# Moving the chunk-recurrence steps by one dense group: levels at groups 0, 3, 5, 8 of ten, preparation ahead of the near sums, six weight splits later

## The chip, the cores and the metric

One core of a Trainium2 chip. The time is device microseconds of one launch of the kernel. The kernel before took 1499.67 us in the median of three runs (1497.66 to 1500.48). The execution that was profiled took 1501.16 us; the span of its records is 1499.0 us. TensorE's granted clock has two levels, 1.2 and 2.4 GHz; the mean granted clock of this execution was 0.994 of full speed.

## The reference

Three parts, one after the other, all in float32:

```python
# 1: gated linear attention, B=4, H=8, S=768, D=48
for t in range(S):
    state = alpha[:, :, t, :, None] * state + k[:, :, t] (outer) v[:, :, t]
    y[:, :, t] = einsum('bhd,bhde->bhe', q[:, :, t], state)
x = y.transpose(0, 2, 1, 3).reshape(3072, 384)
# 2: gated layer, d_ff 1536
x = (sigmoid(x @ w_gate) * (x @ w_val)) @ w_out
# 3: four experts of width 1024, each over all tokens
p = domain_probs / domain_probs.sum(-1)
out = sum(p[:, e] * (relu(x @ w1[e]) @ w2[e]) for e in range(4))
```

The recurrence over t is replaced by chunks of 128 tokens. Every float32 product of parts 2 and 3 is made of three products of halves (high x high, high x low, low x high), so each operand is split into a high half, a copy rounded by ScalarE, and a low half, the difference, which VectorE or GpSimd computes.

## The kernel before, in words

**Steps.** A step (`sc`) is one chunk of 128 tokens of one batch entry, 24 in all. Its work on TensorE is a sequence of tasks. Six levels (`LVL`, level 0 to 5, products of K columns with the Q columns in `QX`, L565, at the last level L568) double the reach within the chunk: 16 matmuls of 64 columns each, at level 5 eight. Then come a transpose of k (`TRK`, L573), the output and state products (`YOUT`, `STATE`, L584 to L596) and a transpose of y (`TRX`, L601), which makes the chunk a part of the next dense tile's input. Between two levels of one step lies a chain: VectorE multiplies Q and K by decays (`move_on`, L882) once the level's products are done; ScalarE copies Q columns into `QX` for the next level (`spread_heads`, two instructions of L772); then TensorE may run the next level. For levels 0 to 2 VectorE also keeps the products (L937), for levels 3 to 5 ScalarE does (L743, L749, ahead of its copies of L772).

**Preparation.** Before level 0 of a step VectorE runs `prepare` (L891, L893, L897: a product of decays, and Q and K multiplied), then ScalarE `spread_heads(..., 0)`. GpSimd computes the further decays (L1074) from the result of L891. The task `PREP` stands for this. Each step's inputs (`A`, `KQ`) are loaded by SyncE's queue (L481, L482) into one of two buffers once the step before the last is done with it (`y_done`, `state_done`, `y_near_ready`).

**Near terms.** Beside the levels, GpSimd multiplies rows (`near_products`, L1081 to L1084), VectorE sums them (`near_sums`, L909), and GpSimd makes a part of the output of them (`near_terms`, L1091, L1097), which VectorE adds to y (L947). The row loads of the next step wait for the near terms.

**Dense tiles.** Part 2 runs over 8 tiles of 384 tokens. A tile is a list of 36 groups of nine matmuls of 384 columns, in the order gate f, value f, out f-1. Behind a gate group ScalarE takes the sigmoid (L785), behind a value group VectorE multiplies (L974), ScalarE takes the high half (L789) and GpSimd the low half (L1114), which the out group of the same f needs.

**The order.** Every engine walks the same list: `attention_slots` puts the tasks of the next tile's three steps into the slots of the groups, and each engine does its part of a slot's tasks ahead of its part of the group. In tiles 2 to 7 task number n of 12 stands at group n * 30 // 12, that is at 0, 2, 5, 7 of every ten groups: level 3 of the running step at 0 (with `PREP` of the next), level 4 with the next step's level 0 at 2, level 5 with level 1 at 5, y, state and the next step's level 2 at 7, `TRX` two groups behind. In the first tile (`FIRST_SLOTS`) the tasks stand at every second group. The last tile has no steps. The first three steps run ahead of the first tile (`FIRST`). Banks of the accumulation memory are given out in turn over the same order of tasks.

**Weights of part 2.** The nine pieces n (gate, value, out for each third of the width) are loaded at the start and split: high halves on ScalarE (`high_raw1`, L820, 128x1536), low halves on GpSimd for n = 0 to 2 and 6 to 8 (L1130, L1136), on VectorE for n = 3 to 5 (L989, one third or fourth of a piece at a time). The second third of the weights is needed from gate 4 (group 9 of the first tile) on, the last from gate 8 (group 21) on. ScalarE splits pieces 3 to 5 between the tasks of `FIRST`, and pieces 6 to 8 behind groups 3, 5, 7 of the first tile; VectorE's ten parts stand behind groups 0 to 9, GpSimd's ten behind groups 2, 4, ... 20.

Part 3 starts at about 700 us and uses neither steps nor these splits.

Of the kernel before, what the change touches and what calls it, by code (L numbers as in the profile page):

```python
# [38 lines left out]
CHUNKS = S // C  # L39
# [11 lines left out]
STEPS_T = T1 // C  # L51
# [21 lines left out]
PREP = "prepare"  # L73
AHEAD = 3
ATT_GROUPS = 30


def attention_slots(first_tile):


    slots = [[] for _ in range(ATT_GROUPS + 3)]
    lead = AHEAD if first_tile else 0

    def at(n):
        return 2 + 2 * (n + lead) if first_tile else n * ATT_GROUPS // (4 * STEPS_T)

    if first_tile:
        slots[0].append((PREP, 0, 0))
    for n in range(lead):
        slots[at(n - lead)].append((LVL, 0, n))  # L90
    for n in range(4 * STEPS_T):
        tasks = []
        for j in range(STEPS_T + 1):
            level = n - 4 * j + AHEAD
            if level == LEVELS:
                tasks += [(YOUT, j, 0), (STATE, j, 0)]
        for j in range(STEPS_T + 1):
            level = n - 4 * j + AHEAD
            if 0 <= level < LEVELS:
                tasks.append((LVL, j, level))  # L100
            if level == 0:
                slots[at(n) - 2].append((PREP, j, 0))
            if level == LEVELS - 1:
                slots[at(n) + 1].append((TRK, j, 0))
            if level == LEVELS:
                slots[at(n) + 2].insert(0, (TRX, j, 0))
        slots[at(n)] += tasks
    return slots
# [29 lines left out]
def buffer_of(i, sc):  # L138

    return sc if is_first(i, sc) else sc % 2  # L140
# [95 lines left out]
def attention_moe_program(nc, qk, alpha, v, rows, w_gate, w_val, w_out, probs, w1, w2, masks, eye, out):  # L236
    with ExitStack() as ctx:
# [483 lines left out]
        def _(act):  # L721
            def task(i, base, kind, j, level):
# [2 lines left out]
                if not in_use(kind, sc) or not exists(i, sc):  # L725
                    return
                if kind == PREP:
                    spread_heads(i, sc, 0)
                    return
                bank = PS[:, att_bank0 + bank_of((kind, j, level), base), :]  # L730
                if kind == LVL and level >= MASKED:
# [30 lines left out]
            def spread_heads(i, sc, level):  # L762


                p = buffer_of(i, sc)
                if level == 0:
                    act.wait_ge(prep_ready, per_step(i, sc, 1, 1))
                else:
                    act.wait_ge(kq_ready[p], per_level(i, sc, level - 1))
                for g, rows in enumerate((slice(0, D), slice(HB, HB + D))):  # L770
                    right = level_columns(KQ[p][rows, 0], level)
                    done = nc.scalar.activation(QX[p][rows, :, g, :].rearrange("d a (n t) -> d a n t", t=2 << level), right, ACT.Copy)  # L772
                done.then_inc(qx_ready[p], 1)

            def next_columns(i, base, kind, j, level):


                if kind == LVL and level < LEVELS - 1 and exists(i, base + j):
                    spread_heads(i, base + j, level + 1)

            def group(i, tc, kind, f):
                if kind == "gate":
# [13 lines left out]
            def tile(i, tc, attend=True, follow=True, between={}, ahead=None):  # L796
                slots = slots_of(i, tc) if attend else []
                for n, (kind, nxt, f) in enumerate(dense_groups(follow)):
                    if ahead and (kind, f) == ("out", FC1 - 1):
                        ahead()  # L800
                    for t in slots[n] if n < len(slots) else []:
                        task(i, STEPS_T * (tc + 1), *t)
                    for t in slots[n] if n < len(slots) else []:
                        next_columns(i, STEPS_T * (tc + 1), *t)
                    group(i, tc + nxt, kind, f)
                    if n in between:
                        between[n]()
# [11 lines left out]
                act.wait_ge(raw1_in[n % RAW1], 16 * (n // RAW1 + 1))  # L819
                nc.scalar.activation(weight_parts(n)[0], raw_piece(n), ACT.Copy).then_inc(weight_high, 1)  # L820

            high_after = {(LVL, 0, 2): 0, (LVL, 0, 3): 1, (LVL, 0, 4): 2, (STATE, 0, 0): 3, (TRX, 0, 0): 4, (STATE, 1, 0): 5}
            spread_heads(0, 0, 0)
            spread_heads(0, 1, 0)
            for t in FIRST:
# [5 lines left out]
                    high_raw1(high_after[t])  # L831
            group(0, 0, "gate", 0)
            group(0, 0, "value", 0)
            tile(0, 0, between={2 * n - 9: (lambda n=n: high_raw1(n)) for n in (6, 7, 8)})
            tile(0, 1)
            with act.Fori(1, B - 1) as i:
                tile(i, 0)
# [29 lines left out]
        def _(dve):  # L867
# [44 lines left out]
            def task(i, base, kind, j, level):  # L912
                sc = base + j
                p, chunk = buffer_of(i, sc), sc % CHUNKS
                if not in_use(kind, sc) or not exists(i, sc):
                    return
                if kind == PREP:
                    prepare(i, sc, 0)
                    prepare(i, sc, 1)
                    return  # L920
                bank = PS[:, att_bank0 + bank_of((kind, j, level), base), :]
                if kind == LVL:
# [15 lines left out]
                                            bank.rearrange("s (g n r) -> s g n r", g=H, r=r)).then_inc(level_kept[p], 1)  # L938
                    if is_first(i, sc):
                        first_decays(sc, level)  # L940
                    if base and level == 3:
                        near_sums(i, sc)
                elif kind == YOUT:
                    wait_count(dve, trx_done, per_step(i, sc, 1, 0))
                    dve.wait_ge(y_near_ready, per_step(i, sc, 1, 1))
# [63 lines left out]
                    near_sums(0, sums_after[t])  # L1009
            group(0, 0, "value", 0)  # L1010
            parts = [(n, k) for n in (3, 4, 5) for k in range(THIRD if n == 5 else KD)]
            tile(0, 0, between={at: (lambda n=n, k=k: low_part1(n, k)) for at, (n, k) in enumerate(parts)})

            dve.wait_ge(prob_in, 16)
            dve.tensor_reduce(psum_e[:], prob[:], AX.X, ALU.add).then_inc(prob_step, 1)
# [48 lines left out]
        def _(pool):  # L1064
# [114 lines left out]
            near_products(0, STEPS_T)  # L1179
            group(0, 0, "value", 0)  # L1180
            parts = [(n, k) for n in (6, 7, 8) for k in range(THIRD if n == 8 else KD)]
            tile(0, 0, between={2 + 2 * at: (lambda n=n, k=k: low_part1(n, k)) for at, (n, k) in enumerate(parts)})
            tile(0, 1)
            with pool.Fori(1, B - 1) as i:
                tile(i, 0)
# [76 lines left out]
```

## Time and profile before

| | |
|---|---|
| median of three runs | 1499.67 us |
| profiled execution, its span | 1501.16 us, 1499.0 us |
| TensorE busy | 1435.9 us, 96% of the span |
| VectorE, ScalarE, GpSimd busy | 603.1, 501.4, 583.6 us |
| start-up (first three steps) | 0 to 52 us |
| part 2 with steps beside it | 52 to about 650 us |
| part 3 | from about 700 us |

The busy shares of the slower engines say little: they work in short chains between the matmuls. What counts is where TensorE stands still, so the views below are its waits and the timeline of single steps. Ends of matmuls are modelled and overlap the next start, so distances between starts are the better measure.

### The profile page before, as it was taken

The page shows a single profiled execution, that of the slowest core. Times are in us where ns is not written, and L with a number is a line of the kernel's source. Part 1 is how long each engine was busy: PE and PEld are TensorE (multiplying, and loading weights), DVE is VectorE, ACT ScalarE, POOL GpSimd, SP SyncE. Part 2 cuts the span into 40 slices and gives each one's busy share as a digit, 9 for nine tenths or more (in the row PEclk, how much of TensorE's full clock was granted, in tenths as well). Part 3 has the DMA queues.
Part 4 walks back from the last instruction along what each step waited for, and adds up shares of the span by engine and source line. Part 5 has one row for each costly group of instructions (what it writes and reads, how often), then busy time and mean ns, then how long its engine had stood idle before and what let it go on. Part 6 is the DMA issues. An engine that isn't in the chain of part 4 may idle for free.

```text
span 1499.0 us, 25799 instructions
## 1 busy us (share of the span) xinstructions
PE 1435.9 (96%) x10296; PEld 1324.3 (88%) x10296; DVE 603.1 (40%) x933; ACT 501.4 (33%) x975; POOL 583.6 (39%) x552
## 2 busy tenths in 40 slices
PE   4889999999999999999999999999999999999999
PEld 4888898998889998999999999999999999999998
DVE  7665554536454545312333333333333333333333
ACT  6654534445444445322222222222222222222220
POOL 6574544534454435254423313323234133242120
PEclk9999999999999999999999999999999999999999
DMA  8322221212121212100001001010010010100011
GB/s 302 113 77 76 82 70 51 94 58 83 52 70 51 101 51 83 43 22 22 0 1 43 0 1 42 0 42 1 0 42 0 0 42 0 42 0 0 17 46 63
DMA packets 31109, 70.65 MB, mean 47 GB/s; under 512 B 5168, under 2 KB 14128, under 8 KB 31024
## 3 DMA queue, kind: packets, MB, share of 16 engines
q1 hardware_dynamic: 31024, 69.43, 13.6%
q8 instruction: 64, 1.05, 0.3%
q14 instruction: 21, 0.17, 0.0%
HBM read 64.70 MB, written 4.72 MB: 46 GB/s over the span
## 4 chain that ended last, share of the span: by engine, by line
PE 89%; DVE 4%; ACT 3%; issue 2%; DMA 1%; SPq 0%; DVEq 0%; ACTq 0%
PE PS L671 27%; PE PS L661 27%; PE PS L617 18%; PE PS L627 9%; PE PS L565 4%; ACT QX L772 2%; PE PS L588 2%; DVE near L909 1%; PE PS L584 1%; DVE KQ L897 1%; DMA raw<-in_w_gate 1%; PE PS L568 1%; DVE KQ L882 1%; PE PS L573 1%; DVE TOT L891 0%
## 5 line engine op out<-in xcount | busy, mean ns | idle before, releaser
L1145 POOL TENSOR_TENSOR XS_0l<-x2T,XS_0h 128x1536 fp32r<-128x1536 f32 x24 | 84.5, 3523 | 263.3 <-ACT XS_0h L815 263.3
L1035 DVE SCALAR_TENSOR_TENSOR acc<-PS,prob,acc 128x384 f32<-128x384 f32 x192 | 118.6, 618 | 161.8 <-PE PS L671 161.8
L1145 POOL TENSOR_TENSOR XS_1l<-x2T,XS_1h 128x1536 fp32r<-128x1536 f32 x23 | 80.8, 3514 | 252.4 <-ACT XS_1h L815 252.4
L772 ACT ACTIVATE QX<-KQ 48x256 f32<-48x256 f32 x288 | 120.4, 418 | 151.1 <-DVE KQ L882 103.3
L856 ACT ACTIVATE H_1h<-PS 128x512 fp32r<-128x512 f32 x96 | 57.5, 599 | 311.7 <-PE PS L661 311.7
L856 ACT ACTIVATE H_0h<-PS 128x512 fp32r<-128x512 f32 x96 | 57.3, 600 | 299.4 <-PE PS L661 299.3
L1043 DVE SCALAR_TENSOR_TENSOR H_1l<-PS,H_1h 128x512 fp32r<-128x512 f32 x96 | 66.4, 692 | 197.0 <-ACT H_1h L856 197.0
L1043 DVE SCALAR_TENSOR_TENSOR H_0l<-PS,H_0h 128x512 fp32r<-128x512 f32 x96 | 66.1, 691 | 188.8 <-ACT H_0h L856 188.8
L565 PE MATMUL PS<-QX,KQ 112*64 112x64 f32 x1920 | 81.7, 237 | 56.3 <-ACT QX L772 55.8
L565 PEld LDWEIGHTS PS<-QX,KQ 112*64 112x64 f32 x1920 | 71.8, 148 | 70.5 <-issue 41.0
L882 DVE TENSOR_TENSOR KQ<-KQ,TOT 112x512 f32<-112x512 f32 (+1 forms) x126 | 103.0, 840 | 75.4 <-PE PS L565 48.7
L974 DVE TENSOR_TENSOR hid<-PS,hid 128x384 f32<-128x384 f32 x96 | 53.4, 557 | 164.6 <-PE PS L617 144.4
L1114 POOL TENSOR_TENSOR hs1l<-hid,hs1h 128x384 fp32r<-128x384 f32 x48 | 51.9, 1082 | 130.1 <-ACT hs1h L789 130.1
L1114 POOL TENSOR_TENSOR hs0l<-hid,hs0h 128x384 fp32r<-128x384 f32 x48 | 53.4, 1113 | 106.7 <-ACT hs0h L789 106.7
L785 ACT ACTIVATE hid<-PS 128x384 f32<-128x384 f32 x96 | 47.2, 492 | 80.1 <-PE PS L617 79.1
L937 DVE COPY_PREDICATED AT<-mask,PS 128x512 f32<-128x512 int32 x72 | 65.9, 916 | 0.5
L671 PE MATMUL PS<-W_0l,H_1h 128*128 128x384 f32 x192 | 65.0, 339 | 0.0
L671 PE MATMUL PS<-W_0h,H_0l 128*128 128x384 f32 x192 | 64.9, 338 | 0.0
L671 PE MATMUL PS<-W_0h,H_1l 128*128 128x384 f32 x192 | 64.9, 338 | 0.0
L671 PE MATMUL PS<-W_0l,H_0h 128*128 128x384 f32 x192 | 64.8, 338 | 0.0
L671 PE MATMUL PS<-W_1l,H_0h 128*128 128x384 f32 x192 | 64.8, 337 | 0.0
L671 PE MATMUL PS<-W_0h,H_0h 128*128 128x384 f32 x192 | 64.8, 337 | 0.0
(157 smaller groups left out, 4117.0 us busy)
## 6 DMA issues: line engine op xcount, KB each, us to landing
row<-in_rows SPq DMA_DIRECT2D x24, 768.0 KB, 4.4
KQ<-in_qk SPq DMA_DIRECT2D x24, 448.0 KB, 4.3
V<-in_v SPq DMA_DIRECT2D x24, 384.0 KB, 4.9
rawA<-in_w SPq DMA_DIRECT2D x8, 768.0 KB, 4.6
rawB<-in_w SPq DMA_DIRECT2D x8, 768.0 KB, 6.3
A<-in_alpha SPq DMA_DIRECT2D x24, 224.0 KB, 2.8
out_y<-acc SPq DMA_DIRECT2D x5, 768.0 KB, 3.5
raw<-in_w_gate SPq DMA_DIRECT2D x3, 768.0 KB, 13.2
```

The lines of the kernel that those rows point to most:

```text
L565: mm = pe.matmul(dst[mine, :, right], KQ[p][0:R, 1, a, mine], cols[:, :, right], start=True, stop=True)
L617: mm = pe.matmul(PS[:, bank, 0:T1], W[w][:, n, f * P:(f + 1) * P], xT[p][x][:, n, :], start=(n == 0 and (w, x) == SPLITS[0]), stop=(n == K ...
L627: mm = pe.matmul(PS[:, out_bank0 + n, 0:T1], WO[w][:, f, n * P:(n + 1) * P], hs[f % 2][x][:], start=(f == 0 and (w, x) == SPLITS[0]), stop ...
L661: mm = pe.matmul(PS[:, hidden_banks[f], :], W1[c // TILES2][w][:, n, f * P:(f + 1) * P], XS[c % 2][x][:, n, :], start=(n == 0 and (w, x) = ...
L671: mm = pe.matmul(PS[:, result_banks[u], 0:DM], H2[c % 2][x][:, f, u * P:(u + 1) * P], W2[c // TILES2 % 2][w][:, f, :], start=(f == 0 and ( ...
L772: done = nc.scalar.activation(QX[p][rows, :, g, :].rearrange("d a (n t) -> d a n t", t=2 << level), right, ACT.Copy)
L856: nc.scalar.activation(H2[c % 2][0][:, f, :], PS[:, hidden_banks[f], :], ACT.Relu).then_inc(rh_ready, 1)
L882: dve.tensor_tensor(x, x, y, ALU.mult).then_inc(kq_ready[p], 1)
L1035: dve.scalar_tensor_tensor(out=acc[:, n, :], in0=PS[:, result_banks[u], 0:DM], scalar=weight, in1=acc[:, n, :], op0=ALU.mult, op1=ALU.add) ...
L1043: dve.scalar_tensor_tensor(out=low, in0=PS[:, hidden_banks[f], :], scalar=0.0, in1=high.bitcast(F32), op0=ALU.max, op1=ALU.subtract).then_ ...
L1114: nc.gpsimd.tensor_tensor(hs[f % 2][1][:], hid[f % 2][:], hs[f % 2][0][:].bitcast(F32), ALU.subtract).then_inc(hl_ready, 1)
L1145: nc.gpsimd.tensor_tensor(XS[c % 2][1][:], x2T[:, :, at:at + T2], XS[c % 2][0][:].bitcast(F32), ALU.subtract).then_inc(xsl_ready, 1)
```

## The change

The positions of the twelve task numbers in tiles 2 to 7 become 0, 3, 5, 8 of every ten groups. `PREP` keeps its slot there and in the first tile, but the work behind it changes place: ScalarE's copies for the next step's level 0 move behind all tasks of the slot and behind the running step's copies for level 4, and VectorE's near sums of the running step move from ahead of `prepare` to behind it. The high halves of pieces 3 to 8 are all made in the first tile, behind groups 1, 3, 5, 7, 9, 11; VectorE's parts stand behind groups 2 to 11, GpSimd's behind groups 9, 10, 11, 13, 14, 15, 17, 18, 19, 20.

```diff
     def at(n):
-        return 2 + 2 * (n + lead) if first_tile else n * ATT_GROUPS // (4 * STEPS_T)
+        return 2 + 2 * (n + lead) if first_tile else n // 4 * (ATT_GROUPS // STEPS_T) + (0, 3, 5, 8)[n % 4]
...
             if level == 0:
-                slots[at(n) - 2].append((PREP, j, 0))
+                slots[at(n - 1)].append((PREP, j, 0))
...
@@ ScalarE @@
                 if kind == PREP:
-                    spread_heads(i, sc, 0)
                     return
...
                 if kind == LVL and level < LEVELS - 1 and exists(i, base + j):
                     spread_heads(i, base + j, level + 1)
+                elif kind == PREP and exists(i, base + j):
+                    spread_heads(i, base + j, 0)
...
-            high_after = {(LVL, 0, 2): 0, (LVL, 0, 3): 1, (LVL, 0, 4): 2, (STATE, 0, 0): 3, (TRX, 0, 0): 4, (STATE, 1, 0): 5}
+            high_after = {(LVL, 0, 2): 0, (LVL, 0, 3): 1, (LVL, 0, 4): 2}
...
-            tile(0, 0, between={2 * n - 9: (lambda n=n: high_raw1(n)) for n in (6, 7, 8)})
+            tile(0, 0, between={2 * n - 5: (lambda n=n: high_raw1(n)) for n in range(3, 9)})
...
@@ VectorE @@
+                if kind == PREP:
+                    if exists(i, sc):
+                        prepare(i, sc, 0)
+                        prepare(i, sc, 1)
+                    if not (isinstance(i, int) and CHUNKS * i + sc == STEPS_T):
+                        near_sums(i, sc - 1)
+                    return
                 if not in_use(kind, sc) or not exists(i, sc):
-                    return
-                if kind == PREP:
-                    prepare(i, sc, 0)
-                    prepare(i, sc, 1)
                     return
...
-                    if base and level == 3:
-                        near_sums(i, sc)
...
-            tile(0, 0, between={at: (lambda n=n, k=k: low_part1(n, k)) for at, (n, k) in enumerate(parts)})
+            tile(0, 0, between={at: (lambda n=n, k=k: low_part1(n, k)) for at, (n, k) in enumerate(parts, 2)})
...
@@ GpSimd @@
-            tile(0, 0, between={2 + 2 * at: (lambda n=n, k=k: low_part1(n, k)) for at, (n, k) in enumerate(parts)})
+            tile(0, 0, between={9 + at + n - 6: (lambda n=n, k=k: low_part1(n, k)) for at, (n, k) in enumerate(parts)})
```

## Rows read from the trace of the kernel before

**Rows 1.** Busy time by stretch: stretch, its length, TensorE busy (instructions), granted clock, DMA share, GB/s.
```profile
145.00:650.00 505.00, 475.99 (x4738) 0.99 0.19 66
700.00:1499.00 799.00, 796.09 (x3992) 1.00 0.05 18
```

**Rows 2.** TensorE's waits, 52 to 145 and 145 to 650 us: total us, times, longest.
```profile
PE PS L565 <- ACT QX L772: 7.7, 5, 2.3
...
PE PS L565 <- ACT QX L772: 28.5, 17, 1.8
```

**Rows 3.** Timeline of TensorE: start, duration, then the idle time before and its releaser.
```profile
79.19 1.42 PE L565 MATMUL PS<-QX,KQ 112*64 112x64 f32 x32 [2.31 <-ACT QX L772]
...
102.33 1.15 PE L565 MATMUL PS<-QX,KQ 112*64 112x64 f32 x32 [2.15 <-ACT QX L772]
...
125.64 1.15 PE L565 MATMUL PS<-QX,KQ 112*64 112x64 f32 x32 [2.30 <-ACT QX L772]
```

**Rows 4.** Timeline of TensorE: first dense matmul behind a level 3.
```profile
231.37 0.44 PE L617 MATMUL PS<-xT0h,WGh 128*128 128x384 f32 x1
```

**Rows 5.** Chain of waits: two dense groups on end (start, us, what).
```profile
239.27 3.12 PE PS L617 x18
```

**Rows 6.** Timeline of VectorE in the same step.
```profile
231.49 0.69 DVE L882 TENSOR_TENSOR KQ<-KQ,TOT 112x512 f32<-112x512 f32 x1 [1.56 <-PE PS L565]
232.10 0.94 DVE L909 TENSOR_REDUCE near<-row 128x16 f32<-128x768 f32 x1
232.96 0.41 DVE L891 TENSOR_TENSOR TOT<-A 112x256 f32<-112x256 f32 x1
...
233.90 0.62 DVE L897 TENSOR_TENSOR KQ<-KQ,TOT 112x256 f32<-112x256 f32 x1
```

**Rows 7.** Timeline of ScalarE in the same step.
```profile
231.95 1.09 ACT L749 ACTIVATE AT<-PS 16x128 f32<-16x128 f32 x4
234.55 1.73 ACT L772 ACTIVATE QX<-KQ 48x256 f32<-48x256 f32 x4 [1.51 <-DVE KQ L897]
```

**Rows 8.** Timeline of ScalarE ahead of the first tile's first pair.
```profile
74.38 1.47 ACT L820 ACTIVATE WOh<-raw 128x1536 fp32r<-128x1536 f32 x1
75.76 1.09 ACT L749 ACTIVATE AT<-PS 16x128 f32<-16x128 f32 x4
```

**Rows 9.** TensorE by stretch, from the start of three pairs on: columns as in rows 1.
```profile
102.33:108.30 5.97, 5.97 (x50) 0.71 0.00 0
...
201.23:208.77 7.54, 7.54 (x60) 0.77 0.47 158
...
236.33:242.32 5.99, 5.99 (x59) 1.00 0.01 3
```

**Rows 10.** Level 2 of a step on TensorE, and ScalarE's copies for its level 3.
```profile
543.76 0.65 PE L565 MATMUL PS<-QX,KQ 112*64 112x64 f32 x16
...
547.04 0.85 ACT L772 ACTIVATE QX<-KQ 48x256 f32<-48x256 f32 x2 [5.33 <-DVE KQ L882]
```

**Rows 11.** Behind a pair: copies at 236.33's, moves and copies at 79.19's.
```profile
238.68 1.72 ACT L772 ACTIVATE QX<-KQ 48x256 f32<-48x256 f32 x4
...
79.98 4.32 DVE L882 TENSOR_TENSOR KQ<-KQ,TOT 112x512 f32<-112x512 f32 x2 [1.78 <-PE PS L565]
...
84.33 0.85 ACT L772 ACTIVATE QX<-KQ 48x256 f32<-48x256 f32 x2 [0.58 <-DVE KQ L882]
```

**Rows 12.** Level 2 behind the state, the load's issue, and its landing (page, part 6).
```profile
249.12 0.65 PE L565 MATMUL PS<-QX,KQ 112*64 112x64 f32 x16
...
249.99 0.33 SPq L482 DMA_DIRECT2D KQ<-in_qk  x1
...
KQ<-in_qk SPq DMA_DIRECT2D x24, 448.0 KB, 4.3
```

**Rows 13.** GpSimd by stretch in the first tile, and its weight parts (groups by line).
```profile
76.80:102.00 25.20, 18.11 (x24) 0.93 0.23 76
...
L1136 POOL TENSOR_TENSOR WVl<-raw,WVh 128x512 fp32r<-128x512 f32 x3 | 3.8, 1284 | 0.0
```

## The prediction

> **What bounds the kernel now.** I read the busy time by stretches first. From 700 us to the end TensorE is busy for 796.09 of 799.00 us: nothing the diff touches can be won there, that part only starts earlier or later. From 145 to 650 us, the tiles in which attention steps run beside the dense layers, it is busy for 475.99 of 505.00, so 29.0 us are idle [rows 1]. Next come the waits of TensorE: 28.5 of those 29.0 us are one kind, 17 waits of L565 (the level products) for the ScalarE copies of L772 (QX), none longer than 1.8; the first tile has five more of that kind, 7.7 us [rows 2]. The timeline shows where: always the pair of 32 matmuls, level 4 of the running step and level 0 of the next. In the first tile these pairs waited 2.31, 2.15 and 2.30 [rows 3].
>
> Then one such step in full. The 16 matmuls of level 3 start in group 0 and the dense matmuls behind them at 231.37 [rows 4]. A group of nine takes 1.56 us (18 in 3.12) [rows 5], so two groups end at 234.49; the pair starts only at 236.33, where the last window of [rows 9] begins. On VectorE meanwhile: move_on of level 3 (L882) at 231.49, the near sums (L909) at 232.10, then the three operations of prepare, the first at 232.96, the last at 233.90 and done at 234.52 [rows 6]. ScalarE ends its level 3 copies at 233.04, idles 1.51 us for prepare, and runs four copies of L772 from 234.55 to 236.28 [rows 7]: first two for the next step's level 0, then two for the running step's level 4. The chain is level 3, near sums, prepare, next step's copies, own copies, level 4. It is a latency chain that two groups of dense work don't cover.
>
> **The change part by part.** The numbers 0 to 35 are dense groups of a tile.
>
> Three groups instead of two behind level 3 (groups 0 to 3, 10 to 13, 20 to 23), near sums behind prepare, own copies first. In the step above: three groups end at 231.37 + 3 x 1.56 = 236.05. Prepare starts where the near sums did, 232.10, and lasts as before 1.56 (232.96 to 234.52), so it ends at 233.66 [rows 6]. The copies of L772 take 1.73 / 2 = 0.865 a step [rows 7]: the running step's run from 233.04 to 233.91, the next step's to 234.77. Both are in by 236.05 with 1.3 us to spare, and the second is only needed half a pair later (1.15 / 2 = 0.58 [rows 3]). All 17 waits go: **-28.5 us**. What hides the chain then is the third dense group; without it, the other two edits alone would bring 0.86 (near sums, by the starts 232.10 and 232.96), 0.865 and 0.58, 2.3 in all, against a wait of 1.8 at most, so they too nearly do it. The wait has two covers.
>
> In the first tile the distance stays two groups; only near sums and order change, worth those 2.3 us. The waits of 2.15 and 2.30 go: -4.45. The one of 2.31 at 79.19 goes in part, because there ScalarE is late itself: a weight copy (L820) runs until 75.85 and the level 3 copies until 76.85 [rows 8]. The own copies then end at 77.7 where TensorE comes at 79.19 - 2.31 = 76.88, and the next step's at 78.6 where the first half of the pair ends at 78.3: 0.85 + 0.3 remain, **-1.15**. Together -5.6.
>
> The clock. Four times the granted clock fell behind such a wait, from 2.4 to 1.2 GHz for a part of the window: twice in the first tile (the one from 102.33, 0.71 granted, stands for both) and twice later (that from 201.23, 0.77 granted, for both: 7.54 us passed for what takes 5.99 at 1.00) [rows 9]. Each costs 1.55 us. Ahead of each, TensorE had stood idle for the wait. Of the later two both go, -3.1. Of the first tile's, the one at 102.33 goes, -1.55; the one at 79.19 I leave, as a wait is left there. Bounds: 0 and -6.2.
>
> What is shortened. Level 4 to level 5 has groups 3 to 5, two where it had three; level 2 to level 3 has 8 to 10, two for three. Level 2 first, one of its latest rows: the level 2 products start at 543.76, and ScalarE has the copies for level 3 at 547.04 + 0.85 = 547.89, 4.13 later [rows 10]. The products (0.65), two groups (3.12) and the transposes of y (0.25, an estimate: three matmuls twice as wide as the sixteen of 0.65) cover 4.02. The excess is 0.11. It applies at 12 places (two in each of six tiles; behind the third stands the tile's end). Allowing for a few later ones I take **+0.5** in all; the upper bound, 19, is worked out under rival 2. Level 4 to 5: the level 1 copies behind the pair of 236.33 end at 240.40, 4.07 after its start [rows 11]; there are 1.15 + 3.12 and 0.5 for level 5, which goes ahead of level 1: 4.8. I take 0, upper bound 20 by the same rival.
>
> The next step's inputs. PREP of group 10 refills a buffer that is free once Y and STATE of group 8 (before: 7) are done. Its KQ load was issued at 249.99, 0.9 behind the state products (level 2 follows them at 249.12), and a load lands after 4.3 us (median) [rows 12]: 5.2 behind them. Prepare will come level 2, two groups, transposes, level 3 and move_on later, 0.65 + 3.12 + 0.25 + 0.65 + 0.69 = 5.36. So this transfer, hidden before, becomes just hidden, and a delay of up to 1.3 us more is taken by the spare time above. Cost 0, upper bound a few tenths for each of 12 places. SyncE's queue issues nothing else in another order. On GpSimd decays, near terms and near products keep their order; each is released earlier relative to its step. VectorE's gating product (hid) of group 7 now stands ahead of the Y work rather than behind it, which can only help the output groups.
>
> The weights. Three ScalarE copies of 1.47 (L820 [rows 8]) leave the start-up stretch before the first tile, where the last step's work on VectorE ends last; I take 0 (bounds one copy, -1.5, and 0). In the first tile copy 3 now stands in group 1, ahead of level 0's copies, which TensorE needs hardly later than they came: **+0.1**, bounds 0 and +1.47. VectorE's parts move two groups back and GpSimd's ten parts are pressed into groups 9 to 20: that is a rival.
>
> **The sum** against the profiled execution (1501.16, span 1499.0): -28.5 - 3.1 - 4.45 - 1.15 - 1.55 + 0.5 + 0.1 = -38.15, so 1463.0. The median of the timed runs is 1.5 below that execution: 1461.5, given as **1462**.
>
> **Rivals.**
> 1. GpSimd becomes the bound in the first tile. From 76.8 to 102 it was busy 18.11 of 25.20 us; four more weight parts of 1.28 fall into the stretch, and the stretch shrinks by some 4 us: 23.2 of 21 [rows 13]. Its low halves (hs) stand behind the parts in the queue and the output groups wait for them. Against it: such a low half has about three groups until it is needed. Price 5 us and a fall of the clock, 1.55: 1468 to 1469. Chance 0.1.
> 2. The two-group distances stall. For it: an L882 takes 0.69 [rows 6], but a pair of them took 4.32 instead of 1.4 where GpSimd had much to do; the copies for level 1 ended at 85.18 there, 5.99 after the pair's start at 79.19 [rows 11], 1.2 more than the 4.8 there are. At 17 places this is 20 us. One L882 stretched by half as much, 1.47, on the 0.11 of level 2 makes 19 at 12 places. Against it: that row is from the first tile, with weight parts on GpSimd. If half of it comes, 19 us are given back: 1481. Chance 0.16. The Trainium skill ("SBUF — State Buffer", "SBUF: two separate sides") has the rule that speaks for this: VectorE operations with two SBUF inputs and GpSimd operations take a shared port pair by an exclusive lock, and the loser waits for the whole instruction. By that rule each new coincidence costs VectorE the rest of one GpSimd operation. The trace agrees: L882 is stretched where GpSimd had a part of 1.28 us and more under way [rows 13].
> 3. Slower. The same mechanism at full strength at all 29 places (39 us), because the new distances set VectorE's moves regularly beside GpSimd's near terms and near products, and with the idle time more falls of the clock at 1.55. It decides from 29 stalls of 1.3 us on, just the saving of 38: with two falls more, 1503 to 1505. Chance 0.05.
> 4. Nothing changes: the inputs of the step (KQ) land so late at the 12 places where the buffer comes free in group 8 that what is won elsewhere is lost there. That wants landings 1.3 + 38 / 12 = 4.5 us behind the median. 1500. Chance 0.03.
>
> **How the numbers follow.** Forecast 0.66 (its own range 1458 to 1468), rivals 0.1, 0.16, 0.05, 0.03. The low end is all idle and slow-clock time of this kind gone, 28.5 + 7.7 + 6.2 + 1.5 = 43.9: 1456. The high end, 1480, is rival 2 at about half strength; beyond lie rivals 3 and 4 and the upper half of 2. A measurement of this kernel tells 0.2% (3 us) from no change. Faster 0.92, within 0.2% 0.03, slower 0.05.
>
> **What would show it.** Right: no L565 wait for QX from 145 us on; a granted clock of 1.00 throughout that stretch; L909 behind L897; the second half starting 38 us earlier, and its length unchanged. Wrong: waits of L565 x16 (level 3) or L568 (level 5) for QX would be rival 2; waits of L627 for the low halves between 75 and 100 us rival 1; VectorE's L891 idle for KQ rival 4.

## The result, and the profile after

The changed kernel takes 1462.16 us (median of 4 runs, 1461.55 to 1463.24), the kernel before 1498.66 beside it (1497.6 to 1500.48): a ratio of 0.9756, 95% interval 0.9739 to 0.9773. The profiled execution took 1463.24, its span is 1461.3. In this trace the lines have moved: L883 is the old L882 (move_on), L892 to L898 are prepare (old L891 to L897), L910 is near_sums (old L909), L771 the copies of QX (old L772), L748 the products that ScalarE keeps (old L749), L991 and L1138 the weight parts of VectorE and GpSimd (old L989, L1136), L1076 GpSimd's decays (old L1074).

The page of the changed kernel, its first part and the shares of the chain:

```profile
PE 1430.0 (98%) x10296; PEld 1319.9 (90%) x10296; DVE 609.7 (42%) x933; ACT 501.2 (34%) x975; POOL 584.0 (40%) x552
...
PE 94%; DVE 2%; ACT 2%; issue 1%; DMA 1%; SPq 0%; DVEq 0%; ACTq 0%
```

TensorE's busy time by stretches (columns as in [rows 1]):

```profile
52.00:145.00 93.00, 87.25 (x868) 0.97 0.24 76
145.00:650.00 505.00, 504.25 (x4918) 1.00 0.20 68
...
662.50:1461.30 798.80, 795.89 (x3991) 1.00 0.05 18
```

Of the 29.0 us idle between 145 and 650 us [rows 1], 0.75 are left, at a granted clock of 1.00. The second half is as long as it was. TensorE's waits over the whole span (line <- releaser: us, times, longest):

```profile
PE PS L565 <- ACT QX L771: 23.1, 14, 7.7
...
PE PS L573 <- DVE KQ L883: 0.6, 1, 0.6
```

All 14 of these waits stand ahead of 145 us, eight of them in the start-up; six (4.7 us) lie between 52 and 145, and the 17 of [rows 2] are gone. One step of tile 3 shows how. TensorE's rows (start, duration, instruction) are the level 3 products, the last dense matmul of the third group, and the pair:

```profile
219.05 0.69 PE L565 MATMUL PS<-QX,KQ 112*64 112x64 f32 x16
...
224.31 0.34 PE L627 MATMUL PS<-hs0h,WOl 128*128 128x384 f32 x1
224.58 1.15 PE L565 MATMUL PS<-QX,KQ 112*64 112x64 f32 x32
```

VectorE's rows behind that level 3:

```profile
219.78 0.69 DVE L883 TENSOR_TENSOR KQ<-KQ,TOT 112x512 f32<-112x512 f32 x1 [1.56 <-PE PS L565]
220.39 0.42 DVE L892 TENSOR_TENSOR TOT<-A 112x256 f32<-112x256 f32 x1
220.73 0.69 DVE L894 TENSOR_TENSOR KQ<-KQ,A 112x512 f32<-112x512 f32 x1
221.33 0.62 DVE L898 TENSOR_TENSOR KQ<-KQ,TOT 112x256 f32<-112x256 f32 x1
221.88 0.94 DVE L910 TENSOR_REDUCE near<-row 128x16 f32<-128x768 f32 x1
```

And ScalarE's:

```profile
220.25 1.09 ACT L748 ACTIVATE AT<-PS 16x128 f32<-16x128 f32 x4
221.36 1.74 ACT L771 ACTIVATE QX<-KQ 48x256 f32<-48x256 f32 x4
```

Near sums now stand last. The four copies run back to back and end at 223.10, 1.5 us ahead of the pair; before, they ended where the pair started [rows 7].

### The profile page after: what moved, and what is told of

It is laid out like the page before. It is cut to its first block, busy times and chain, and to the rows that moved or that the text cites. A ratio compares the mean times of both kernels' runs of the same rounds, so it can differ in the third digit from the quotient of the medians.

```text
span 1461.3 us, 25799 instructions
## 1 busy us (share of the span) xinstructions
PE 1430.0 (98%) x10296; PEld 1319.9 (90%) x10296; DVE 609.7 (42%) x933; ACT 501.2 (34%) x975; POOL 584.0 (40%) x552
## 3 DMA queue, kind: packets, MB, share of 16 engines
q8 instruction: 64, 1.05, 0.3%
## 4 chain that ended last, share of the span: by engine, by line
PE 94%; DVE 2%; ACT 2%; issue 1%; DMA 1%; SPq 0%; DVEq 0%; ACTq 0%
PE PS L671 28%; PE PS L661 27%; PE PS L617 21%; PE PS L627 10%; PE PS L565 4%; PE PS L588 2%; PE PS L584 1%; PE PS L568 1%; DMA raw<-in_w_gate 1%; ACT QX L771 1%; PE PS L573 1%; DVE KQ L883 0%; PE PS L596 0%; PE PS L601 0%; ACT AT L748 0%
## 5 line engine op out<-in xcount | busy, mean ns | idle before, releaser
L771 ACT ACTIVATE QX<-KQ 48x256 f32<-48x256 f32 x288 | 120.7, 419 | 130.2 <-DVE KQ L883 107.4
L883 DVE TENSOR_TENSOR KQ<-KQ,TOT 112x512 f32<-112x512 f32 (+1 forms) x126 | 110.7, 902 | 46.0 <-PE PS L565 27.9
```

What stands on the lines that cost most here:

```text
L883: dve.tensor_tensor(x, x, y, ALU.mult).then_inc(kq_ready[p], 1)
```

## Where the 37.7 us came from

I cut both spans (1499.0 and 1461.3) at the first dense matmul and at the first gate product of tile 2.

| stretch | before | after | difference | predicted |
|---|---|---|---|---|
| to the first dense matmul | 51.92 | 50.44 | -1.5 | 0 |
| first tile | 90.55 | 87.44 | -3.1 | -7.05 |
| all the rest | 1356.5 | 1323.4 | -33.1 | -31.1 |

The total was met because three differences nearly cancel: +3.95, -2.0 and -1.5. The last is put down to chance: 1.2 of it is there at the 32 matmuls near 32 us, ahead of anything that changed, and over the 14 profiles of this study the first dense matmul started anywhere from 49.80 to 53.47, in no order that follows the edits.

**The rest.** The prediction took a wait at the idle time that the view gives. From the start of the last dense matmul to the start of the pair it was 2.02 us before (mean of the 17 pairs, 34.27 us in all) and is 0.27 now, so a wait cost 1.75, where the view counts 28.5 / 17 = 1.68; the idle is counted from a modelled end. With 17 x 1.75 = 29.7 and the two falls of the clock at 1.55, 32.8 of the 33.1 are there. The +0.5 for level 3 did not come. One of the later such steps, with ScalarE's copies first and then the level 2 and level 3 products on TensorE:

```profile
240.01 0.84 ACT L771 ACTIVATE QX<-KQ 48x256 f32<-48x256 f32 x2 [3.28 <-DVE KQ L883]
```

```profile
237.37 0.65 PE L565 MATMUL PS<-QX,KQ 112*64 112x64 f32 x16
...
241.60 0.69 PE L565 MATMUL PS<-QX,KQ 112*64 112x64 f32 x16
```

The copies end 3.48 behind the start of level 2, and 0.75 before level 3; behind group 20 it was 0.26 (263.86 and 264.12). The 4.13 of [rows 10] was not carried over.

**The first tile** did not give what was forecast. Three windows from its start on:

```profile
50.44:60.11 9.67, 8.06 (x37) 0.82 0.74 194
60.11:65.62 5.51, 5.51 (x34) 0.69 0.00 0
65.62:69.59 3.97, 3.97 (x36) 1.00 0.00 0
```

Behind a wait of 1.61 the granted clock fell from 2.4 to 1.2 GHz for part of the window 60.11 to 65.62, and 5.51 us passed for about as many matmuls as took 3.97 in the next. The first window has a fall too, as the dense work begins; the kernel before has one at the same place (its row comes first below), and the prediction, which counted falls behind waits for QX, left it out:

```profile
51.92:57.00 5.08, 5.08 (x20) 0.66 1.01 267
```

```profile
50.44:55.00 4.56, 4.56 (x17) 0.63 1.01 255
```

So the first tile had three falls before (the others are the two of the prediction) and has two now. The larger waits that are left:

```profile
60.11 0.69 PE L565 MATMUL PS<-QX,KQ 112*64 112x64 f32 x16 [1.61 <-ACT QX L771]
...
78.29 0.69 PE L565 MATMUL PS<-QX,KQ 112*64 112x64 f32 x16 [0.70 <-ACT QX L771]
...
84.64 0.69 PE L565 MATMUL PS<-QX,KQ 112*64 112x64 f32 x16 [0.84 <-ACT QX L771]
87.73 0.57 PE L573 MATMUL PS<-ident,KQ 112*128 112x112 f32 x4 [0.62 <-DVE KQ L883]
...
101.80 0.69 PE L565 MATMUL PS<-QX,KQ 112*64 112x64 f32 x16 [1.12 <-ACT QX L771]
```

The one of 0.70, with 0.22 in the middle of its pair, is the one of 2.31 before: 0.92 is left where 1.15 was forecast. The first and the last trace back to prepare. VectorE at 56 us, between the two at 80 and 86, and at 98:

```profile
55.95 1.15 DVE L892 TENSOR_TENSOR TOT<-A 112x256 f32<-112x256 f32 x1
57.02 1.50 DVE L894 TENSOR_TENSOR KQ<-KQ,A 112x512 f32<-112x512 f32 x1
...
79.50 4.12 DVE L883 TENSOR_TENSOR KQ<-KQ,TOT 112x512 f32<-112x512 f32 x2
...
86.08 3.20 DVE L883 TENSOR_TENSOR KQ<-KQ,TOT 112x512 f32<-112x512 f32 x2
...
98.10 1.51 DVE L892 TENSOR_TENSOR TOT<-A 112x256 f32<-112x256 f32 x1
```

GpSimd over the same times:

```profile
55.81 1.01 POOL L1086 TENSOR_TENSOR row<-row 128x384 f32<-128x384 f32 x1
56.78 1.19 POOL L1116 TENSOR_TENSOR hs0l<-hid,hs0h 128x384 fp32r<-128x384 f32 x1
...
95.12 4.21 POOL L1138 TENSOR_TENSOR WVl<-raw,WVh 128x512 fp32r<-128x512 f32 x3
```

The L892 that takes 0.42 in the steady tiles takes 1.15 and 1.51 here, and L894 1.50 instead of 0.69, each time beside a run of GpSimd operations: prepare is longer by 1.5 at 56 us and by 1.1 at 98. The waits of 0.84 and 0.62 follow from two pairs of move_on that took 4.12 and 3.20. The first of these pairs is not new: before it took 4.32 [rows 11], but TensorE was 2.31 late by then and did not have to wait for it. The prediction had this row and used it only for rival 2; with the wait ahead of it shortened, it became the next limit.

The long prepare at 56 us is not the change's doing. The near products start when V lands, prepare 5.5 us behind the first dense matmul in these profiles. In the profile of before they came 2.74 behind that matmul and ended as prepare began: its L891 took 0.42, and the wait there was 0.68. In both profiles of the changed kernel they came 3.3 to 3.4 behind it, and the waits were 1.61 and 1.51; in e1_positions, whose order of work here is that of before, the wait was 1.47 with an L891 of 0.99. In all eight profiles other than before's in which step 3 is prepared at this place with full near products, the wait was 1.47 to 2.04. So 0.9 us of wait, and perhaps the fall of the clock behind it, came or stayed away with the start-up of the execution, and the profile of before was the exception.

The wait of 1.12 at 101.80, on the other hand, is the weights' doing. The change puts three of GpSimd's parts behind groups 13 to 15, and prepare of this step runs into them. In the four profiles with the new places and otherwise full work at this place (the change twice, e6_two_apart, e8_early) L892 took 1.51 and the wait was 1.12 to 1.13; in the four that have the new order and the old places (e2_order, e5_weights_old, e10_early_old, e11_early_late8) it took 0.42 and there was no wait. The wait of 0.62 for L883 goes with it: 0.62 to 0.64 in the same four, none in the other four. VectorE's row in e5_weights_old:

```profile
94.93 0.42 DVE L892 TENSOR_TENSOR TOT<-A 112x256 f32<-112x256 f32 x1
```

## Experiments

Each row: median of the timed runs, ratio to the kernel before as timed beside it (1499.63 for e1 to e4, 1500.08 for e5, e6, e8 and e9, 1500.77 for the others), and from the profile the length of the first tile with its mean granted clock, and of the rest.

| kernel | us | ratio, 95% | first tile, clock | rest |
|---|---|---|---|---|
| before | 1498.66 | 1 | 90.55, 0.94 | 1356.5 |
| the change | 1462.16 | 0.9756 [0.9739, 0.9773] | 87.44, 0.96 | 1323.4 |
| e1_positions | 1480.09 | 0.9867 [0.9850, 0.9884] | 93.13, 0.93 | 1335.2 |
| e2_order | 1464.31 | 0.9766 [0.9750, 0.9782] | 82.46, 1.00 | 1326.0 |
| e3_near_only | 1484.63 | 0.9908 [0.9886, 0.9930] | 86.46, 0.98 | 1342.8 |
| e4_copies_only | 1470.53 | 0.9801 [0.9784, 0.9817] | 84.94, 1.00 | 1331.2 |
| e5_weights_old | 1460.96 | 0.9741 [0.9727, 0.9754] | 82.88, 1.00 | 1323.6 |
| e6_two_apart | 1465.45 | 0.9762 [0.9749, 0.9776] | 86.01, 0.98 | 1326.1 |
| e7_light_near | 1458.77 (one run) | | 81.94, 0.98 | 1323.5 |
| e8_early | 1462.29 | 0.9742 [0.9728, 0.9755] | 83.27, 1.00 | 1323.7 |
| e9_early_spread | 1465.48 | 0.9766 [0.9753, 0.9780] | 89.42, 0.94 | 1323.2 |
| the change again | 1461.70 | 0.9744 [0.9727, 0.9761] | 86.09, 0.98 | 1323.9 |
| e10_early_old | 1458.48 | 0.9719 [0.9702, 0.9736] | 81.80, 1.00 | 1323.8 |
| e11_early_late8 | 1459.62 | 0.9728 [0.9712, 0.9744] | 81.84, 1.00 | 1323.8 |

The last two columns are of one execution each; in the two profiles of the changed kernel the rest agrees within 0.5 us (1323.4 and 1323.9), the first tile within 1.4.

**e1_positions**, the distances alone, on the kernel before:

```diff
-        return 2 + 2 * (n + lead) if first_tile else n * ATT_GROUPS // (4 * STEPS_T)
+        return 2 + 2 * (n + lead) if first_tile else n // 4 * (ATT_GROUPS // STEPS_T) + (0, 3, 5, 8)[n % 4]
```

> Only the positions 0, 3, 5, 8 of the change; near sums, copies and weights as before. Theory (two covers, each nearly enough alone): the copies for level 4 end at 236.28 in the step of the trace before, three groups at 236.05, so each of the 17 waits shrinks from 1.68 to 0.2 or 0.3 us. The first tile keeps its 7.7 us of waits and its falls of the clock. 17 x 1.45 + 3.1 (clock) = 27.8: about 1471, 1468 to 1474. Rival (the order of near sums and copies does nearly all): 10 us or more slower than that, 1480. Rival (two-group distances stall at levels 5 and 3): waits of L565 x16 or L568 for QX, over 1476.

1480.09: 9 us above what was expected, and where the rival had it. The stretch and its waits, in this kernel:

```profile
145.00:650.00 505.00, 493.48 (x4862) 1.00 0.21 68
```

```profile
PE PS L565 <- ACT QX L772: 10.8, 15, 1.5
```

And the pair behind groups 0, 10 and 20 of a tile:

```profile
154.95 1.15 PE L565 MATMUL PS<-QX,KQ 112*64 112x64 f32 x32 [0.24 <-ACT QX L772]
...
177.45 1.15 PE L565 MATMUL PS<-QX,KQ 112*64 112x64 f32 x32 [0.59 <-ACT QX L772]
...
201.47 1.15 PE L565 MATMUL PS<-QX,KQ 112*64 112x64 f32 x32 [1.44 <-ACT QX L772]
```

The waits are graded by the step's place in the tile. VectorE says what is late, in a step at group 20 whose level 3 products start at 273.64:

```profile
275.13 0.56 DVE L967 TENSOR_TENSOR xT1l<-PS,xT1h 128x384 fp32r<-128x384 f32 x1 [1.03 <-ACT xT1h L759]
275.61 0.76 DVE L882 TENSOR_TENSOR KQ<-KQ,TOT 112x512 f32<-112x512 f32 x1
```

With the new distances the transposes of the next tile's input (TRX) come in the group where level 3 comes. Their low half, which waits for ScalarE's high half, then stands ahead of move_on in VectorE's queue: move_on starts 1.97 behind level 3, and 0.74 behind it where the step is at group 0 (227.88 and 228.62). At group 10 ScalarE's half is in time, and it is 1.15 (250.51 and 251.66). That eats up most of the 1.56 that the third group brings. The idle time between 145 and 650 still falls from 29.0 to 11.5, less than half of it.

**e2_order**, the other two edits without the distances (near sums behind prepare, own copies first; both below):

> Only the order: near sums behind prepare on VectorE, own copies ahead of the next step's on ScalarE; positions 0, 2, 5, 7 and weights as before. Theory (two covers): worth up to 0.86 + 0.865 + 0.58 = 2.3 us per wait, so the 17 waits of 1.68 and those of 2.15 to 2.3 in the first tile all but go: 1460 to 1465, as fast as the whole change within 3 us. Rival (the third group is what counts, the order is a by-work): a half of each wait stays, 17 x 0.8 = 14 us, 1475 or more.

1464.31, as expected, and within 2 us of the whole change, which was timed beside another set of runs. Its stretch and its waits there:

```profile
145.00:650.00 505.00, 503.60 (x4904) 1.00 0.21 68
```

```profile
PE PS L565 <- ACT QX L771: 0.4, 2, 0.2
```

What it lacks to the change is the second half of some pairs. TensorE behind group 21:

```profile
266.53 0.34 PE L617 MATMUL PS<-xT0h,WGl 128*128 128x384 f32 x1
266.80 1.52 PE L565 MATMUL PS<-QX,KQ 112*64 112x64 f32 x32
```

The pair starts in time, but takes 1.52 instead of 1.15: the level 0 products still wait for the next step's copies. It is so in five of the 17 pairs, always the third of a tile, 1.85 us in all from start to start; the two longest stops are the waits of 0.2 above. With three groups every pair takes 1.15. So the distances are worth 1326.0 - 1323.4 = 2.6 us of the rest once the order is right, and 21.3 (1356.5 - 1335.2) without it.

**e3_near_only** moves only the near sums, and **e4_copies_only** only the copies:

```diff
                 if kind == PREP:
...
+                    if not (isinstance(i, int) and CHUNKS * i + sc == STEPS_T):
+                        near_sums(i, sc - 1)
...
-                    if base and level == 3:
-                        near_sums(i, sc)
```

```diff
                 if kind == PREP:
-                    spread_heads(i, sc, 0)
                     return
...
+                elif kind == PREP and exists(i, base + j):
+                    spread_heads(i, base + j, 0)
```

> Only the near sums of the running step moved behind prepare, all else as before. Theory: the chain is near sums, prepare, next step's copies, own copies, so each of 20 waits loses 0.86 us, 17 us, and with shorter waits perhaps one to three falls of the clock at 1.55: 1478 to 1482. Rival (VectorE and GpSimd get into each other's way where prepare now lies, so part of it is lost): 1485 or more.

> Only the running step's copies moved ahead of the next step's on ScalarE, all else as before. Theory: level 4 no longer waits for prepare (its copies end at 233.9, two groups at 234.5), and level 0 waits for copies that end at 235.4 where TensorE comes at 235.1: each wait falls from 1.68 to about 0.4, 17 x 1.3 + 3 x 1.3 = 26 us, and 3 of clock: 1468 to 1473. So the copies' order alone is worth more than the near sums alone. Rival (the two are worth 0.86 each, equal): 1480.

1484.63 for the first (1481.22 to 1488.6), some 3 us above what was expected; its waits between 145 and 650 fall from 1.68 to 1.05 each (17.8 in 17), where the prediction had 0.86 for this edit. The mean hides two kinds: in the first two steps of a tile 0.69 to 0.95 is left, in the third 1.50 to 1.68, nearly all. There prepare, now earlier, runs beside GpSimd, and its L893 took 1.50 in all five such steps instead of 0.69, so the rival that was named for this run is what happened in one step of three:

```profile
269.73 1.50 DVE L893 TENSOR_TENSOR KQ<-KQ,A 112x512 f32<-112x512 f32 x1
```

```profile
269.49 1.20 POOL L1115 TENSOR_TENSOR hs1l<-hid,hs1h 128x384 fp32r<-128x384 f32 x1 [3.76 <-ACT hs1h L789]
270.65 2.45 POOL L1075 TENSOR_TENSOR TOT<-TOT 112x128 f32<-112x128 f32 x6
```

1470.53 for the second, as expected; 3.0 us of waits are left in 13 pairs, the longest 0.33. The two do not add: -15 and -29 apart, -35 together, since the wait was about 1.7 and there is no more to take. The second edit also takes prepare, stretched or not, off the path of level 4. The copies are the main part, for they do more than the 0.865 that the prediction put on them: they take near sums, prepare and the other copies out of the way of the pair's first half altogether, which then hangs only on level 3 and its own copies.

**e5_weights_old**, the whole change but with the first tile's weight copies and parts where they were:

```diff
-            high_after = {(LVL, 0, 2): 0, (LVL, 0, 3): 1, (LVL, 0, 4): 2}
+            high_after = {(LVL, 0, 2): 0, (LVL, 0, 3): 1, (LVL, 0, 4): 2, (STATE, 0, 0): 3, (TRX, 0, 0): 4, (STATE, 1, 0): 5}
...
-            tile(0, 0, between={2 * n - 5: (lambda n=n: high_raw1(n)) for n in range(3, 9)})
+            tile(0, 0, between={2 * n - 9: (lambda n=n: high_raw1(n)) for n in (6, 7, 8)})
```

> The whole change but for the weights: the six pieces are split where they were before. Theory (the weight move is worth nothing measurable): the first tile's waits are as long as with it, 3.8 us (seen in the run with the order alone) against 3.7 with the whole change: 1461 to 1465. Rival (the weight move takes ScalarE's and VectorE's work out of the way of the first steps): 1466 or more. Rival (pressing GpSimd's parts together costs): below 1461.

1460.96 (1459.05 to 1462.67), where the change has 1461.70 and 1462.16: just below the expected range, at the edge of the rival that pressing GpSimd's parts together costs. The timed runs can't tell it from nothing; the profiles can in part. The first tile is shorter without the move (82.88 against 87.44 and 86.09); much of that is the clock, which did not fall in this execution, but TensorE's idle time, which leaves the clock out, is 4.64 against 5.75 and 5.88. e8_early and e10_early_old, which again differ in the weights alone, have 4.50 and 3.30. So the move costs the first tile some 1.1 to 1.2 us of idle time, by the waits of 1.12 and 0.62 above less what it saves at 79 us.

**e6_two_apart**, the change with two groups behind level 3 everywhere:

```diff
-(0, 3, 5, 8)[n % 4]
+(0, 2, 4, 6)[n % 4]
```

> The whole change with positions 0, 2, 4, 6 instead of 0, 3, 5, 8, so every level is two groups behind the one before, and four groups lie ahead of the next level 3. Theory (with the new order a distance of two groups is long enough everywhere): 1461 to 1466, with single short waits where the transpose of k and the state products are one group apart. Rival (two groups aren't enough where VectorE and GpSimd meet): at 29 places waits of 0.5 us and more, 1475 or more.

1465.45, as expected, and one wait of 0.2 between 145 and 650; four of the 16 pairs that start and end without a wait take 1.49 to 1.50. The rest (1326.1) is that of e2_order. In tiles 2 to 7 two groups are enough for every level; this ends rival 2, which had them stall there.

**e7_light_near** is the change with GpSimd's near products and near terms computed for one head of eight (48 of 384 columns) in all but the first steps; the near terms of the other heads are left out.

```diff
-                nc.gpsimd.tensor_tensor(row[:, 1], row[:, 1], row[:, 0], ALU.mult).then_inc(qa_ready, 1)
+                nc.gpsimd.tensor_tensor(row[:, 1, 0:to], row[:, 1, 0:to], row[:, 0, 0:to], ALU.mult).then_inc(qa_ready, 1)
```

> The changed kernel with most of GpSimd's near work left out: near products and near terms are computed for one head of eight (48 of 384 columns), for all steps with the outputs' near parts accordingly missing. Theory (VectorE's moves are stretched by GpSimd operations beside them): the mean of L883 falls from 902 to 720 to 780 ns and pairs of 2.4 us in the steady tiles become 1.3; the time stays within 2 us of 1462 outside the first tile's gain, since TensorE no longer waits: 1459 to 1463. Rival (the stretch has another cause): the mean stays near 900.

VectorE's move_on, on the page of this kernel and then on that of the change (busy, mean ns of one | idle):

```profile
L883 DVE TENSOR_TENSOR KQ<-KQ,TOT 112x512 f32<-112x512 f32 (+1 forms) x126 | 91.9, 751 | 50.3 <-PE PS L565 26.9
```

```profile
L883 DVE TENSOR_TENSOR KQ<-KQ,TOT 112x512 f32<-112x512 f32 (+1 forms) x126 | 110.7, 902 | 46.0 <-PE PS L565 27.9
```

The same 126 instructions fall from 902 to 751 ns (720 to 780 were expected) with nothing changed on VectorE, so GpSimd's work stretches them. In the steady tiles this costs TensorE nothing (504.32 of 505.00 busy against 504.25). In the first tile the near products now end at 54.68, prepare's L892 and L894 take 0.41 and 0.69, and the wait of 1.61 is 0.67; the others are 0.71, 0.22 and 0.16, that of 1.12 is gone with an L892 of 0.42 there, and the tile is 4.2 to 5.5 us shorter than in the two profiles of the change. The Trainium skill ("SBUF — State Buffer", "SBUF: two separate sides") has the rule: VectorE operations with two SBUF inputs and GpSimd share a port pair under an exclusive lock. By that rule the traces agree: an operation of 0.42 becomes 1.15 or 1.51 beside GpSimd operations of 1.0 us and of 1.4 (three in 4.21). The lock itself no run shows.

**e8_early, e9_early_spread, e10_early_old, e11_early_late8** look for the first tile's missing gain. All prepare step 3 and copy its heads ahead of the first dense group, where the near products are not yet under way:

```diff
             spread_heads(0, STEPS_T, 0)
             group(0, 0, "gate", 0)
...
             prepare(0, STEPS_T, 0)
             prepare(0, STEPS_T, 1)
             group(0, 0, "value", 0)
```

e8 does this on the change. e9 also spreads VectorE's parts over groups 2 to 9, 12 and 13, and GpSimd's over 11 to 25. e10 is e8 with the old places of the weights (as e5). e11 is e10 with the copies of pieces 6, 7 and 8 behind groups 3, 5 and 11.

> The whole change, and step 3 is prepared (VectorE's three operations, ScalarE's copies for its level 0) ahead of the first dense group instead of in group 0 of the first tile. In the trace of the changed kernel these operations meet GpSimd's near products (1.15 and 1.50 us instead of 0.4 and 0.7), level 0 waits 1.61 us and the clock falls behind it (1.55). Theory: both go, if the inputs of step 3 have landed by 50 us; 2 to 3 us faster than the changed kernel: 1459 to 1460.5. Rival (the inputs land later, and the first groups wait for them): 1462 or more.

> As the run before, and the weight parts of the first tile keep clear of the pairs of levels: VectorE's last two parts behind groups 12 and 13, GpSimd's ten behind groups 11, 14, 15, 17, 19 to 23 and 25. Theory (the first tile's other waits, 3.7 us, come from moves stretched by GpSimd's parts: the pair at 79.50 took 4.12 us): 1 to 2 us faster than the run before, 1457 to 1459. Rival (near terms and decays stretch them as much): no difference, 1459 to 1460.5.

> Positions and order of the change, weights split where they were before, and step 3 prepared ahead of the first dense group. Theory: the wait of level 0 in group 2 (1.9 us in the run with the old weights) goes, half a microsecond comes back as a later sigmoid: 1.3 us faster than that run, 1458.5 to 1461. Rival (only the place of the loss moves): 1461 or more.

> As the run before, and ScalarE's copy of weight piece 8 stands behind group 11 instead of group 7, where it held up the copies for level 4 (a wait of 0.98 there). Theory: this wait goes, 0.5 to 1 us faster than the run before, 1457.5 to 1460. Rival (the stretched moves on VectorE wait there anyway): no difference.

e8: 1462.29, above the expected 1459 to 1460.5. The wait of 1.61 is gone; in its place stands one of 0.5 on TensorE, for ScalarE's sigmoid:

```profile
57.15 0.44 PE L617 MATMUL PS<-xT0h,WGh 128*128 128x384 f32 x1 [0.52 <-ACT hid L786]
```

The first tile is 2.8 to 4.2 us shorter than with the change, but timed runs show none of it. e9: 1465.48, 6 above the range that was expected. Its last prepare meets GpSimd's parts (1.24, 1.49 and 1.21 for the three operations), which makes a wait of 2.48, and the last third of the weights is too late for output group 8, which makes one of 3.35:

```profile
120.69 0.69 PE L565 MATMUL PS<-QX,KQ 112*64 112x64 f32 x16 [2.48 <-ACT QX L771]
...
124.72 0.69 PE L627 MATMUL PS<-hs0h,WOh 128*128 128x384 f32 x1 [3.35 <-POOL WOl L1142]
```

e10: 1458.48 (1457.02 to 1460.14), at the low edge of what was expected, and 3.2 below the change timed beside it (1461.22 to 1464.20): the fastest version here, against the kernel before and, as the two sets of runs do not overlap, against the changed one, though the intervals of the two ratios still touch. Its first tile has 3.3 us of idle time (78.50 of 81.80 busy), the change's 5.75 (81.69 of 87.44) with the clock at 0.96. Between e10 and e5 only the early preparation differs; the 2.5 between them lie across two sets of runs and are not shown to be more than noise. The same holds for the 3.8 between e10 and e8, which differ in the weights. e11: 1459.62, no difference from e10; it traded waits of 0.99, 0.23 and 0.70 for 0.80 and 1.20.

## Why the prediction was right, and where it was wrong

1. **The mechanism was right in tiles 2 to 7.** The chain level 3, near sums, prepare, next copies, own copies, level 4 made the waits; all 17 are gone, L910 stands behind L898, the clock is 1.00 throughout and the second half has its length. That the time, 1462 against 1462.16, is met to 0.2 us is luck: +3.95 and -2.0 -1.5 happened to cancel.
2. **"The wait has two covers" was wrong in one half.** "What hides the chain then is the third dense group" was worked out with the other edits in place; read as a cover of its own, as e1's expectation had it, it fails: alone it leaves 10.8 us in 15 waits (e1), since it also moves TRX ahead of move_on in the steps behind groups 10 and 20 in e1; the prediction followed one step in full and took the others to be alike. The other cover, 0.86, 0.865 and 0.58, "2.3 in all", holds: alone it brings 35 us, and the third group the last 2.6. Its first part does not hold by itself: e3 got 0.63 a wait, and next to nothing in every third step.
3. **The term -4.45 with -1.55 for the first tile was mis-sized.** "The waits of 2.15 and 2.30 go": 1.12 of one stayed, the wait of 0.68 at the tile's start became 1.61, and the total of the tile is -3.1 instead of -7.05. TensorE's idle time fell by 2.4 (8.14 to 5.75), where a fall by 5.6 was forecast, and its busy time by 0.7, where 1.55 was forecast for the clock. The 3.2 of idle time that is missing is four waits: 0.93 more at 60.11, the 1.12, and the new ones of 0.84 and 0.62. The prediction took prepare at the steady 1.56 and the collision of its own profile, or the lack of one, for fixed, and did not carry the move_on pair of 4.32 from its rival into the sum. e7 shows for the first place that GpSimd is what stretches prepare; for the one at 98, the profiles with the new and the old places of the weights do.
4. **+0.5 for level 3 was 0**, with 0.26 and 0.75 to spare in the two steps above. It came from copies that were late before for another reason: level 3 of [rows 10] was measured behind a delayed chain.
5. **The waits were undercounted** by 1.2 (29.7 against 28.5) as a view counts idle time from a modelled end.
6. **The start-up**, taken at 0: nothing there is shown to have changed.
7. **The weights**, "+0.1" with 1.47 as the upper bound: 1.1 to 1.2 of idle time in the first tile, which is within the bound but by another way. The prediction priced ScalarE's copy in group 1; what cost was GpSimd's parts beside VectorE's work. In the timed runs (e5) it does not show.
8. **Rivals.** Rival 1 (GpSimd bound): the mechanism was there in part, as stretched VectorE work and not as late low halves; no L627 wait for hs came. Rival 2 is refuted for tiles 2 to 7 by the change (no wait of that kind) and by e6, rival 3 with it. The stretched pairs exist there, 0.69 to 1.2 an instruction, and more of them than before (the mean of move_on rose from 840 to 902 ns), but they have room. In the first tile, where the distances did not change, the same stretch made the wait of 0.84. Rival 4: the KQ load was issued at 238.25 and prepare ran at 243.36 without waiting for it, so it stays hidden.

Open: whether the slow clock in the first tile belongs to a version. In six profiles (before, both of the change, e1, e7, e9) it fell as the dense work began, with no step's wait ahead of it. Counting all falls of the tile: with the new places of the weights slow clock came in both profiles of the change, in e6, e7 and e9, and not in e8; with the old ones in before, e1 and e3, and not in e2, e4, e5, e10 and e11. One execution each doesn't settle it.

## What to carry to other kernels

On an in-order engine that serves a running step and the next, put what the running step needs first and what no one waits for last; here that alone brought 35 of 37 us, and needs no distance. Greater distance between dependent groups comes after that, and each position moved has to be followed through every queue that it passes in every place of the tile, not in one step of it. A saving worked out at steady durations does not hold where GpSimd is busy beside VectorE: take the durations from that stretch. The same goes for work that no one waits for: three weight parts in a row on GpSimd made a wait of 1.12 through VectorE. And when one wait is cut, look for what it had hidden; here a pair of moves of over 4 us, visible in the rows before, came next.

## What the runs showed of the hardware

- VectorE operations on SBUF operands lengthen beside GpSimd work: 0.42 to 1.15 and 1.51 us (112x256), 0.69 to 1.50 (112x512); the mean of 126 fell from 902 to 751 ns when GpSimd's work was cut.
- The granted clock in the first tile differs between profiles: 0.96 and 0.98 in two executions of the same kernel. Behind a wait of 1.6 us it fell in one profile and cost about 1.5 (5.51 against 3.97); behind a wait of 1.86 (e5) it stayed at 1.00.
- The first dense matmul started between 49.80 and 53.47 us over 14 profiles, which is more than any experiment on the first tile was worth; hence the lengths from mark to mark.
